# Routing each block's tokens during the next dense block, with a list of (token, gate) pairs in DRAM

## What is computed

```python
x   = attention(q, k, v)                    # local window plus a 4x coarser one; then [2304, 512]
h   = x @ w_in;  x = (h * np.cos(h)) @ w_out          # dense layer, 512 -> 2048 -> 512
logits = x @ w_gate                                   # [2304, 8]
expert = argmax(logits, axis=1)
gate   = softmax(logits)[n, expert]
out[n] = gate[n] * (relu(x[n] @ w1[expert]) @ w2[expert])   # 512 -> 1024 -> 512
```

## Time and profile before

| | us |
|---|---|
| median of three runs | 939.99 |
| the profiled execution | 942.13, its span 940.3 |
| PE busy (matmuls) | 844.7 (90%) |
| DVE, ACT, POOL busy | 543.9, 399.2, 338.7 |
| attention, dense layer | 0 to 166, 166 to 613 |
| last dense matmul to first expert matmul | 612.9 to 654.0 |
| a dense block (L911 of chunk 14 to the same of the next block) | 74.0 (455.89 to 529.87) |
| DVE idle before L879 at chunk 15 | 0.41 |
| mean granted TensorE clock | 0.944 of full |

### The profile page before, as it was taken

One profiled execution on the slowest core, in us unless ns is written; L12 is line 12 of the kernel. 1 busy time (PEld: TensorE's weight loads), 2 busy tenths in 40 slices (PEclk: granted clock), 3 DMA queues, 4 the chain that ended last, 5 costly groups with the idle time before them and its releaser, 6 DMA issues.

```text
span 940.3 us, 16363 instructions
## 1 busy us (share of the span) xinstructions
PE 844.7 (90%) x5833; PEld 719.0 (76%) x5834; DVE 543.9 (58%) x835; ACT 399.2 (42%) x686; POOL 338.7 (36%) x440
## 2 busy tenths in 40 slices
PE   3797978789999999999999999943999999999996
PEld 2676766679899798799889889732888888888884
DVE  1888786666656656646646655555634525536521
ACT  2676674443424433433433433340543524525521
POOL 4888885334333334324333333401122112211221
PEclk9869697999999999999999999965999999999998
DMA  9889860200000000000000030035615526336111
GB/s 169 195 182 207 190 138 17 88 24 1 34 1 2 34 0 0 26 8 0 0 33 0 0 123 1 0 124 201 213 61 192 168 87 221 107 139 218 39 38 35
DMA packets 89020, 77.96 MB, mean 83 GB/s; under 512 B 64014, under 2 KB 68622, under 8 KB 88976
## 3 DMA queue, kind: packets, MB, share of 16 engines
q1 hardware_dynamic: 81968, 57.97, 22.8%
q0 software_dynamic: 3680, 11.02, 3.4%
q10 hardware_dynamic: 3328, 8.39, 3.0%
HBM read 67.91 MB, written 10.49 MB: 83 GB/s over the span
## 4 chain that ended last, share of the span: by engine, by line
PE 70%; DVE 17%; ACT 6%; issue 3%; DMA 1%; SPq 1%; POOL 1%; DVEq 0%; ACTq 0%; POOLq 0%
PE psum L1193 17%; PE psum L1207 16%; PE psum L1287 13%; PE psum L1304 13%; DVE angle L908 2%; PE psum L1296 2%; PE psum L1222 2%; DVE angle L905 1%; DVE turns L903 1%; ACT angle L722 1%; PE psum L1275 1%; DVE probs L843 1%; ACT angle L724 1%; DVE max_l L840 1%; DVE sum_l L847 1%
## 5 line engine op out<-in xcount | busy, mean ns | idle before, releaser
L1193 PE MATMUL psum<-x_hi,w_in 128*128 128x384 f32 x768 | 218.7, 345 | 9.5 <-DVE turns L911 8.3
L1207 PE MATMUL psum<-w_out,g_hi 128*128 128x512 f32 x576 | 182.3, 398 | 9.2 <-ACT x L734 6.4
L722 ACT ACTIVATE angle<-angle 128x384 f32<-128x384 f32 x96 | 50.4, 525 | 256.9 <-DVE angle L908 256.9
L565 POOL TENSOR_SCALAR g_hi<-turns 128x384 fp32r<-128x384 f32 x96 | 53.5, 558 | 289.1 <-DVE turns L911 286.7
L1193 PEld LDWEIGHTS psum<-x_hi,w_in 128*128 128x128 f32 x768 | 142.3, 190 | 19.0 <-DVE turns L911 13.1
L1193 PE MATMUL psum<-x_lo,w_in 128*128 128x384 f32 x384 | 130.7, 340 | 0.0
L1207 PEld LDWEIGHTS psum<-w_out,g_hi 128*128 128x128 f32 x576 | 106.8, 189 | 30.3 <-ACT x L734 6.1
L911 DVE TENSOR_TENSOR turns<-angle,psum 128x384 f32<-128x384 f32 x96 | 53.3, 555 | 120.3 <-ACT angle L724 120.3
L1287 PE MATMUL psum<-w,xg_hi 128*128 128x512 f32 x352 | 113.8, 405 | 1.4 <-DVE xg_lo L1027 1.4
L1304 PE MATMUL psum<-w,hT_hi 128*128 128x512 f32 x352 | 114.2, 405 | 0.0
L1207 PE MATMUL psum<-w_out,g_lo 128*128 128x512 f32 x288 | 114.0, 396 | 0.0
(11 more groups left out here) (153 smaller groups left out, 1268.2 us busy)
## 6 DMA issues: line engine op xcount, KB each, us to landing
raw_e<-in_moe_w_dram SPq DMA_DIRECT2D x64, 512.0 KB, 5.9
q_nat<-in_q_dram SPq DMA_DIRECT2D x32, 144.0 KB, 4.2
k_nat<-in_k_dram SPq DMA_DIRECT2D x32, 144.0 KB, 3.9
v_grp<-in_v_dram SPq DMA_DIRECT2D x16, 288.0 KB
x_rows<-x SPq DMA_DIRECT2D x18, 256.0 KB, 2.1
v_win<-in_v_dram SPq DMA_DIRECT2D x64, 70.0 KB
raw<-in_moe_w_in_dram ACTq DMA_DIRECT2D x8, 512.0 KB, 5.4
raw<-in_moe_w_out_dram ACTq DMA_DIRECT2D x8, 512.0 KB, 3.5
```

Source lines behind the costliest of these rows:

```text
L565: pool.tensor_scalar(g_hi[r][:, :], turns[r][:, :], 1.0, 1.0, ALU.mult, ALU.mult).then_inc(ghi_done, 1)
L722: act.activation(angle[r][:, :], angle[r][:, :], ACT.Abs).then_inc(act_step, 1)
L1193: ins = pe.matmul(ps_h[r][:, 0:BT], w_in[:, a, k, cut], x[:, k, :], start=k == 0 and a == 0 and x is x_hi, stop=k == KC - 1 and a == 1)
L1207: ins = pe.matmul(ps_acc[t][:, :], g[r][:, cut], w_out[:, f, a, :], start=f == 0 and g is g_hi and a == 0, stop=f == FC - 1 and g is g_lo)
```

## The change

Routing is done block by block. The slots of each expert are fixed: expert e owns rows 2304 e to 2304 e + 2303 of a DRAM list of (token, gate) pairs, `listed`, so a token's row is known from the counts so far.

- DVE runs `choose` after chunk 8 and `place_rows` after chunk 11 of blocks 1 to 5 for the block before; ACT runs one Exp (`logit_exps`) after chunk 10; PE runs `rank` (five small matmuls) after `accumulate` of chunk 8; POOL scatters three tiles of pairs after chunks 11, 12 and 13, and waits at the block's end until they have landed. The same steps for the last block come after the dense layer. `choose` has seven small DVE instructions on 128 x 24 operands, `place_rows` ten that depend on one another; then, for the last block alone, eight to `tiles_ready` and six to `rows_ready`.
- POOL makes the constants after block 0; SP fills the list with NOBODY once; POOL waits for that before chunk 16.
- The global one-hot matrices, the 18 matmuls L1266 and what follows are gone. Left behind the last block: `choose`, `rank`, `place_rows`, three scatters, tile counts, and for each tile the row of the list at which it begins (`row_i`).
- SP reads each tile's 128 pairs back from DRAM. ACT, DVE and POOL no longer wait for `ids_ready` but for `tiles_ready` (and `list_in`).
- The last block's three tiles have PSUM banks and x2T buffers of their own. All eight pieces of expert 0 are loaded before the last stores. PE waits for the first four pieces at an expert's start and for all eight inside its tile.

```diff
 @block.sync
+            sp.wait_ge(list_blank, 1)
+            sp.dma_start(listed.rearrange("(p n) c -> p (n c)", p=P), no_pairs[:, :]).then_inc(list_empty, 16)
...
+            store_x2(BLOCKS - 1)
+            load_expert(1, range(3))
+            sp.wait_ge(list_stored, 16 * TOK_TILES)
+            sp.wait_ge(rows_ready, 1)
+            def load_pairs(g):
+                at_least(sp, list_in, 16 * g)
+                row = sp.value_load(row_i[0:1, bass.ds(g, 1)], min_val=0, max_val=SLOTS - P)
+                sp.dma_start(pairs_in[:, bass.ds(g, 1), :].squeeze(1), listed[bass.ds(row, P), :]).then_inc(list_in, 16)
+            for g in range(2):
+                load_pairs(g)
+            sp.wait_ge(xg_in, 16)
+            load_expert(1, range(3, PIECES_E))
+            with sp.Fori(2, ID_TILES) as g:
+                load_pairs(g)
+            with sp.Fori(2, E) as e:
+                load_expert(e, range(PIECES_E))
 @block.gpsimd
+            def scatter_rows(done, t):
+                if t == 0:
+                    pool.wait_ge(slot_ready, done)
+                passed(pool, pool_passed)
+                pool.indirect_dma_start(out=listed, out_offset=bass.IndirectOffsetOnAxis(ap=slot_i[:, t:t + 1], axis=0),
+                                        in_=pairs[:, t, :], in_offset=None,
+                                        bounds_check=SLOTS - 1, oob_is_err=False).then_inc(list_stored, 16)
+            pool.wait_ge(list_empty, 16)
+            pool.sem_inc(pairs_free, 1)
             with pool.Fori(1, BLOCKS) as j:
                 for f in range(FC):
                     cut_g(FC * j + f, f % 2)
+                    if 11 <= f < 11 + TT:
+                        scatter_rows(j, f - 11)
+                pool.wait_ge(list_stored, 16 * TT * j)
+                pool.sem_inc(pairs_free, 1)
...
             def gather(g, n):
-                pool.tensor_copy(idx_g[:, :], id_g[:, bass.ds(g, 1)]).then_inc(idx_done, 1)
+                pool.wait_ge(list_in, 16 * g + 16)
+                pool.tensor_copy(idx_g[:, :], pairs_in[:, bass.ds(g, 1), 0]).then_inc(idx_done, 1)
 @block.scalar
+            def logit_exps(done):
+                act.wait_ge(top_ready, done)
+                act.activation(shifted[:, :, :], shifted[:, :, :], ACT.Exp).then_inc(logit_exp, 1)
...
+                    if f == 10 and not (isinstance(j, int) and j == 0):
+                        logit_exps(j)
...
+            act.wait_ge(h_done, FC * BLOCKS)
+            split_e(0, 0, 0)
             evacuate(BLOCKS - 1)
+            for n in range(1, 5):
+                split_e(0, 0, n)
+            logit_exps(BLOCKS)
+            for n in range(5, PIECES_E):
                 split_e(0, 0, n)
 @block.vector
+            def choose(done):
...
+                dve.wait_ge(logits_done, TT * done)
+                then(dve.tensor_reduce(top[:, :], logits, AX_X, ALU.max), 1)
+                dve.tensor_tensor(shifted[:, :, :], logits, per_tile(top[:, :]), ALU.subtract).then_inc(top_ready, 1)
+                then(dve.tensor_tensor(onehot[:, :, :], logits, per_tile(top[:, :]), ALU.is_equal), 2)
...
+                then(dve.tensor_reduce(first[:, :], onehot[:, :, :], AX_X, ALU.max), 4)
+                then(dve.tensor_tensor(onehot[:, :, :], onehot[:, :, :], per_tile(first[:, :]), ALU.is_equal), CHOOSE)
+                dve.tensor_copy(onehot_b[:, :, :], onehot[:, :, :]).then_inc(oh_ready, 1)
+            def place_rows(done):
...
+                dve.wait_ge(logit_exp, done)
+                dve.wait_ge(pairs_free, done)
+                then(dve.tensor_reduce(den[:, :], shifted[:, :, :], AX_X, ALU.add), 1)
+                then(dve.tensor_scalar(den[:, :], den[:, :], 1e-9, None, ALU.add), 2)
+                then(dve.reciprocal(pairs[:, :, 1], den[:, :]), 3)
+                then(dve.tensor_copy(pairs[:, :, 0], tokens[:, :]), 4)
+                then(dve.tensor_scalar(tokens[:, :], tokens[:, :], float(BT), None, ALU.add), 5)
+                dve.wait_ge(ranked, done)
...
+                then(dve.tensor_reduce(slot[:, :], ranks[:, :, :], AX_X, ALU.add), 7)
+                then(dve.tensor_copy(slot_i[:, :], slot[:, :]), 8)
+                dve.sem_inc(slot_ready, 1)
...
+                then(dve.tensor_tensor(seen_b[:, :], seen_b[:, :], block_sum[:, :], ALU.add), PLACE)
+                dve.sem_inc(seen_ready, 1)
...
+                    if f == 8 and not (isinstance(j, int) and j == 0):
+                        choose(j)
+                    if f == 11 and not (isinstance(j, int) and j == 0):
+                        place_rows(j)
...
+            split_e(0, 0, 0)
+            for t in range(TT):
+                dve.wait_ge(x2T_done, TT * (BLOCKS - 1) + t + 1)
+                dve.tensor_copy(x2T_of_end(t), ps_x2T_end[t].rearrange("p (c n) -> p c n", c=KC)).then_inc(x2T_out, 1)
+                if t:
+                    split_e(0, 0, t)
+            choose(BLOCKS)
+            place_rows(BLOCKS)
...
+            dve.sem_inc(tiles_ready, 1)
...
+            dve.sem_inc(rows_ready, 1)
+            for n in range(3, 6):
                 split_e(0, 0, n)
...
             xg_copy(0)
+            for n in range(6, PIECES_E):
+                split_e(0, 0, n)
@block.tensor
+                        if f == 8:
+                            rank(j)
```

More of the change, by code:

```diff
@@ L164, in build @@
         g_lo = [place(f"g_lo{i}", [P, BT], F32R) for i in range(2)]
-        x2 = [place(f"x2_{i}", [P, DM], F32) for i in range(TT)]
+        x2 = place("x2", [P, TT, DM], F32)
         x2T = place("x2T", [P, KC, P], F32)
         assert at[0] >= attention_end
+        x_at = at[0]
         x_hi = place("x_hi", [P, KC, BT], F32R)
@@ new lines, in build @@
+        top = place("top", [P, TT], F32)
+        shifted = place("shifted", [P, TT, E], F32)
+        onehot = place("onehot", [P, TT, E], F32)
+        onehot_b = place("onehot_b", [P, TT, E], BF16)
+        first = place("first", [P, TT], F32)
+        den = place("den", [P, TT], F32)
+        ranks = place("ranks", [P, TT, E], F32)
+        slot = place("slot", [P, TT], F32)
+        slot_i = place("slot_i", [P, TT], I32)
+        block_sum = place("block_sum", [P, E], F32)
+        seen_b = place("seen_b", [P, E], BF16)
@@ new lines, in build @@
+        start_f = place("start_f", [P, E], F32)
+        start_row = place("start_row", [P, E], F32)
+        start_b = place("start_b", [P, E], BF16)
+        iota_e = place("iota_e", [P, E], F32)
+        tokens = place("tokens", [P, TT], F32)
+        before = place("before", [P, P], BF16)
+        ones_b = place("ones_b", [P, P], BF16)
+        ones_f = place("ones_f", [P, E], F32)
+        count_i = place("count_i", [P, E], I32)
+        count_s = place("count_s", [P, E], I32)
+        tiles_f = place("tiles_f", [P, E + 1], F32)
@@ new lines, in build @@
+        upto_f = place("upto_f", [P, E], F32)
+        first_f = place("first_f", [P, E], F32)
+        skip_f = place("skip_f", [P, E], F32)
+        n_tiles = place("n_tiles", [P, E], I32)
+        first_tile = place("first_tile", [P, E + 1], I32)
+        iota_g = place("iota_g", [P, ID_TILES], F32)
+        reached = place("reached", [P, ID_TILES, E], F32)
+        row_f = place("row_f", [P, ID_TILES], F32)
+        row_i = place("row_i", [P, ID_TILES], I32)
+        pairs = place("pairs", [P, TT, 2], F32)
@@ L190, in build @@
[L190 to L199, removed]
@@ L210, in build @@
+        x2T_end = [place(f"x2T_end{i}", [P, KC, P], F32) for i in range(TT - 1)]
         place, at = region(free)
@@ L453, in _ @@
             sp.wait_ge(xs_lo, KC * BLOCKS)
[L455 to L460, removed]
+            for n in range(PIECES_E):
+                if n < KC:
+                    sp.dma_start(raw_e[:, n, :], moe2_w1[0, n * P:(n + 1) * P, :]).then_inc(rawe_in[n], 16)
+                else:
                     c = 2 * (n - KC)
@@ L930, in _ @@
             ff_block(BLOCKS - 1, True)
-            for t in range(TT):
-                x2T_copy(TT * (BLOCKS - 1) + t)
             def split_e(e, par, n):
@@ L1016, in _ @@
-            then(dve.tensor_scalar(empty[:, :], id_f[:, 5, :], -float(NOBODY), float(NOBODY), ALU.mult, ALU.add))
-            then(dve.tensor_tensor(id_s[:, :], id_t[:, :], empty[:, :], ALU.add))
-            then(dve.tensor_tensor(gate_t[:, :], id_f[:, 2, :], id_f[:, 3, :], ALU.add))
-            then(dve.tensor_tensor(gate_s[:, 0:ID_TILES], gate_t[:, :], id_f[:, 4, :], ALU.add))
-            dve.sem_inc(ids_ready, 1)
-            for n in range(2, PIECES_E):
+                dve.wait_ge(rt_end, done[0])
@@ L1215, in x2_turn, with rank, spread_over @@
                 for c in range(KC):
-                    ins = pe.transpose(ps_x2T[:, c * P:(c + 1) * P], x2[t][:, c * P:(c + 1) * P], ident[:, :])
+                    ins = pe.transpose(ps_x2T[:, c * P:(c + 1) * P], x2[:, t, c * P:(c + 1) * P], ident[:, :])
                 ins.then_inc(x2T_done, 1)
+            def rank(done):
+                pe.wait_ge(route_const, 1)
```

(13 more changed lines are left out.)

270 lines of the change are left out of this document (120 added, 150 removed).

## The result

The changed kernel takes 988.8 us (median of 4 runs, 988.17 to 991.67) against 940.11 us beside it: 1.0517 times as long, 95% interval 1.0503 to 1.0531. Forecast: 975, range 952 to 1003. (Two far longer executions of the experiments, 2054.9 and 1088.39 us, are left out of their medians and ranges.) The profiled execution took 988.17 us with a span of 986.4; that of before, 942.13.

| stretch | before | after | change | forecast |
|---|---|---|---|---|
| end of the last dense matmul | 612.88 | 634.81 | +21.9 | +19 |
| from there to the first expert matmul | 41.1 | 29.0 | -12.1 | -15 |
| from there to the end | 286.3 | 322.6 | +36.3 | +29 and +2 |

A forecast was written before the change was run, and what follows sets the result against it. PE was taken to bound the dense layer, with a 41.1 us gap before the experts. 942.1 + 19 (dense) - 15 (gap) + 29 (SP's queue) + 2 (clock) = 977.1 profiled, 975 on the median; range 952 to 1003.

The forecast's parts named there:

- Dense layer: Blocks 1 to 5: routing steps cost 3.8 us a block, 19 us over five blocks; bounds 12 to 22.
- 1.5 us of room: Dense layer's double buffers: DVE may fall 1.5 us behind before PE stops, catching up about 0.15 us a chunk.
- The step with Exp: Dense block, chunk 10: Exp and two table loads make the step 6.2 us, 2.0 more than a chunk.
- PE's two stops: Dense block: 1.1 us beyond the room after the Exp step, then 1.4 us lost to `place_rows`.
- The gap: Last dense to first expert matmul: 26 us instead of 41.1, so 15 less; bounds 11 to 18 less.
- 2.7 to landing: In the gap: each of the last block's three scatters lands 2.7 us after issue, list complete at T+16.
- SP's loop: 25 `load_pairs` rounds of 2.65 us, 66 us, delay expert 2's weights; PE stands 29 us in expert 1, bounds 13 and 58.
- Clock: After the pause in expert 1, a dozen matmuls run at the lowered clock: 2 us more.
- the list does not fit into expert 0: Rival, that it fits: rounds under 1.49 us, no pause in expert 1, 944 us on the median; chance 0.06.
- A mean round of 3.8: Rival: SP's rounds cost 3.8 us and more, stall 58 us, total 1004 us; chance 0.1.
- The gap did close: Rival, that it doesn't: three DRAM landings in a row leave only 3 us gained, 987 us; chance 0.07.
- The drain: Rival: each ACT table switch costs 2.66 us, more than its load; 14 us more, 989 us; chance 0.04.

The follow-up runs named there:

- list in parts: Changed kernel with SP's 25 pair-list reads cut in three (8, 8, 9), expert 2's and 3's weights loaded between; 956.16 us, 1.0138 times before.
- Exp as a copy: Changed kernel with Copy in place of Exp in blocks 1 to 5, so no table loads there; 975.55 us, 1.0379 times before.
- All three: Changed kernel with list reads in three parts, choose and place_rows in DVE's waits, Exp plus a spare sine in ACT's wait; 932.87 us, 0.9925 times before.
- DVE in its waits: Changed kernel with choose and place_rows each halved into DVE's waits (chunks 8, 9, 11, 12), rank and scatters a chunk later; 970.83 us, 1.0319 times before.
- splits after the list: Changed kernel with DVE's splits 3 to 5 of expert 0 put off until the first pairs have landed; 989.89 us, 1.0508 times before.

## Why the prediction was right, and where its terms were off

The case forecast is the case that came: slower, by a pause in expert 1 that SP's queue makes, plus a tax on each dense block, less a shorter gap. The sum was 977.1 for the profiled execution and came out at 988.2. Three terms erred to the same side, the fourth was right, and some 1.6 us at the end had no term:

- **Dense layer, 19 forecast, 21.9 measured.** The mechanism held in each step: 13 ACT_TABLE_LOADs, PE waiting at chunks 13 and 14, 1.5 us of room, nothing lost before it was used up. `choose` was put at 0.95 more than a chunk and took 1.15 (5.35 us less 4.20). I had named the cause and taken a middle value; L1006 lost 0.68 of 0.86 us. The step with Exp was put at 6.2 and took 6.31. `place_rows` was put at 5.6 and took 5.96; its integer conversion L1029 ran 0.43 there, 0.17 at the end of the kernel. PE's two stops are 1.43 and 1.49 in the brackets, forecast 1.1 and 1.4, but cost more: from start to start of the hidden matmuls (L1271) these chunks take 5.80 and 5.96 us for 4.21, 3.3 in all for the 2.5 forecast. `rank` costs 0.2 for 0.4, and at the splits 0.6 is left for 0.85. That is 4.4 us a block (78.4 less 74.0) for 3.8.
- **The gap, 15 less forecast, 12.1 less measured.** Up to the slots I was 0.9 us too slow: POOL's first scatter is issued 9.5 us after the last dense matmul, and I had it at 10.4. The step that failed is "2.7 to landing", taken from out_dram's scatters: the last landed in 6.8. By my working the list would have been complete at T+16; it was at T+19. The rest (2.9 to the pairs on POOL, 7.1 from there to the first expert matmul) was as forecast within half a microsecond.
- **SP's loop, 29 forecast, 32.7 measured.** The loop was entered 3.7 us after the first expert matmul for 2.8. From its first issue to that of expert 2's first piece it took 68.5 for 66: a steady round was forecast well, at 2.65, and took 2.58 (ten of them from 709.30 to 735.13), but the first took 4.96, its read standing behind expert 1's last pieces, and four near 700 us took 3.1 to 3.4. The mean of the 24 is 2.82. That a small read waits for the large ones ahead of it was not in the sum. Expert 2's first piece landed in 3.7 for 3.2. Within the steady round two errors cancelled: the pair tile lands in 1.7 us, not 2.05, and what SP adds around it is 0.9, not 0.6.
- **Clock, 2 forecast, 2.0 measured**, as the step of 47.25 us shows. The other 1.6 of the expert stage's 3.6 lies nearly all behind the last scatter of rows; the sum had nothing for it, and its cause is open.

The rivals: the list does not fit into expert 0 (a round would have to take under 1.49; 2.5 is the least seen). A mean round of 3.8 does not come; single ones behind weights take longer (4.96, and 10.6 in the list in parts). The gap did close. The drain is out by Exp as a copy. That the routing in the blocks is a tax by its place, and not by its work, I had not put among the rivals. All three says it: the same instructions, in the waits of DVE and ACT, cost 1.1 us instead of 21.9 (`rank` and the scatters come a chunk later there).

```profile
270.00:614.00 344.00, 333.14 (x1733) 296.79 (x1731) 222.80 (x411) 143.83 (x271) 134.59 (x164) 1.00 0.06 22
```

That is the dense layer of that kernel, by the columns of the earlier trace rows. DVE does as many instructions as in the changed kernel (411) and PE works 333 of 344 us.

## What to carry to other kernels

Small work moved under a long stage was nearly free here only where it was issued into the waits of the engine it uses; put between two steps of the chain, it used up the double buffer's slack once and was then paid in full. In the rows such a wait is the bracket in front of an instruction (1.24 before L911), and a chain without brackets elsewhere is a sign that what is added will show. And a loop of small dependent transfers ahead of large ones on one queue is priced by rounds times latency: look for the next consumer of that queue, and put its load between the rounds. The round behind that load then waits for all of it (10.6 us here), so its tile must not be the next one needed.

## What was not expected of the hardware

- The longest landing of a scatter was 6.8 us in the changed kernel and 5.4, 5.6, 5.7 and 6.4 in four of the experiments (list in parts, DVE in its waits, splits after the list, all three), with medians of 3.5 to 3.6. It was each time the third of three issued 1.3 us apart. It was not settled why.
- A VectorE instruction of 128x24 took 0.86 us instead of 0.18 beside POOL's g_lo: g_lo ran from 440.11 to 441.13, L1006 from 440.30 to 441.16. It has two SBUF inputs, and its end is g_lo's end within 0.03 us. The rule in the Trainium skill (SBUF — State Buffer, Who interferes with whom) fits this row: it does not run slower, it waits the other one out.
- The clock before the gap is not the same in each run of like code. In the profile of the splits after the list the transposes behind the last dense matmul took 2.82 us for 1.64, and the gap was 32.0 us for 29.0:

```profile
636.61 2.82 PE L1353 MATMUL psum<-ident,x 128*128 128x128 f32 x12 [0.69 <-ACT x L794]
```

  In the list in parts, where the code of the gap is that of the change, the transposes took 2.82 us too and the gap 30.5: a single gap may differ by 1.5 us without a cause in the program. In both of these profiles the first scatter went out 12.4 us after the last dense matmul for 9.5, but the last one landed in 5.7 and 5.4 us for 6.8. Some 1 us of the 32.0 is the edit's own: POOL's index copy L656 ran 1.13 us for 0.19, beside DVE's splits.
